# Four edits around the last batch and the head copies of a fused attention, mixing, Fourier and MLP kernel

## The chip, the cores and the metric

The kernel runs on one core of one Trainium2 chip. The metric is the device time of one launch in microseconds (us). Every product on TensorE is made of 32-bit numbers, most of them split into a high and a low half that TensorE multiplies separately.

## The reference

```python
# attention, batch 4, 8 heads, 576 positions, head width 64
scores = scale * q @ k.T
scores = where(scores >= max(scores) - tau, scores, -1e9)
attn = exp(scores - max); attn /= sum(attn) + 1e-9
x = (attn @ v) as (B, S, 512)
# mixing: xk, xr are x mixed with x one position earlier, by mu_k and mu_r
k = relu(xk @ w_k); v = (k * k) @ w_v; r = sigmoid(xr @ w_r)
x = r * v
# Fourier transform over positions and channels, then an MLP behind a layer norm
u = x + real(fft(fft(x, axis=1), axis=2))
mu = mean(u, -1); var = mean((u - mu) ** 2, -1)
un = (u - mu) / sqrt(var + 1e-6)
out = u + relu(un @ w_ch1) @ w_ch2
```

## The kernel before

The attention is cut into 144 tiles of up to 128 queries, 9 to a pair of heads and 36 to a batch. A slot n of the program works on several tiles at once: TensorE makes the scores of tile n (`qk`, line 816), transposes the probabilities of tile n-3 (line 832) and multiplies those of tile n-4 by v (`pv`, line 849); VectorE takes the row maximum of tile n (line 1350) and masks tile n-1 (line 1361); ScalarE takes the exponential of tile n (line 1092), copies the transposed probabilities of tile n-2 (line 1101) and, where a head ends with tile n-4, copies its output into `x_att`, divided by the row sums (`copy_head`, lines 1114 and 1119). For the first head of a pair that is four copies of 128x64 and two of 64x64 for the tail that both heads share; for the second head it is four copies.

The dense work of a batch (transposes of x, mixing, r, k, v, fold, the transforms y and u) is spread over the 36 slots of the next batch by tables of slots such as `MIX_AT` and `Y_AT`. Each engine has its own list of generators (`mixing`, `dense`), and `run_beside` moves them on once a slot. Every engine runs its instructions strictly in the order in which the program issues them, and waits on semaphores. The last batch (`alone(d)`) has no attention beside it: its dense work alone sets the time there. After it comes an MLP over 5 chunks of 464 columns (`mlp`, `chunk`), with the layer norm of the next chunk prepared beside the current one.

The norm of the first chunk is prepared within the dense work of the last batch. GpSimd adds the four channel tiles of u (`add_tiles`, lines 732 to 739: two sums, their sum, its high half, its low half), TensorE sums over partitions (`mean`, line 855, put behind the first product of stage v), VectorE subtracts the mean (`center`, line 1394), ScalarE squares (line 1261), GpSimd adds the tiles of the squares in the same way, and TensorE makes the variance (`variance`, line 855 again, behind the fourth product of stage v). In between GpSimd makes the low halves of the mixed inputs (`mix_l`, line 685).

The tables of the last transform lie in a scratch tensor in device memory, stored there in slot 34 of the first batch. Each batch loads them into `cs` behind its last product of stage v, the cosines (line 521) and then the sines (line 522), because `cs` shares its place with buffers of stage v. The u groups on TensorE wait for the cosines at g = 0 and for the sines at g = 1 (lines 1003 and 1005). The queue of SyncE issues them between loads of w_1. `u_in` holds two chunks of u; both are loaded early in the last batch.

At the start VectorE makes the high half of k and the low halves of q of the first head: for the first 128 queries (line 1329), then for the other 512 (line 1339). GpSimd makes the low halves of later heads (line 635).

## Time and profile before

| | us |
|---|---|
| median of 3 runs | 1079.55 (1079.39 to 1081.67) |
| the profiled execution | 1079.17 |
| its span | 1077.4 |
| TensorE busy with matmuls | 1053.3 (98%) |
| VectorE busy | 578.3 (54%) |
| ScalarE busy | 511.2 (47%) |
| GpSimd busy | 422.5 (39%) |

The span is the time from the first instruction to the last; the device time of the same execution is 1.8 us longer. Matmuls are pipelined: the profile lets one of 288 columns last 0.30 us, while the next starts 0.13 us after it. A stop of TensorE therefore shows in the starts of neighbouring matmuls, and less, or not at all, in the busy time.

### The profile page before, as it was taken

The page shows a single profiled execution, that of the slowest core. Times are in us where ns is not written, and L with a number is a line of the kernel's source. Part 1 is how long each engine was busy: PE and PEld are TensorE (multiplying, and loading weights), DVE is VectorE, ACT ScalarE, POOL GpSimd, SP SyncE. Part 2 cuts the span into 40 slices and gives each one's busy share as a digit, 9 for nine tenths or more (in the row PEclk, how much of TensorE's full clock was granted, in tenths as well). Part 3 has the DMA queues.
Part 4 walks back from the last instruction along what each step waited for, and adds up shares of the span by engine and source line. Part 5 has one row for each costly group of instructions (what it writes and reads, how often), then busy time and mean ns, then how long its engine had stood idle before and what let it go on. Part 6 is the DMA issues. An engine that isn't in the chain of part 4 may idle for free.

```text
span 1077.4 us, 18500 instructions
## 1 busy us (share of the span) xinstructions
PE 1053.3 (98%) x7088; PEld 1000.4 (93%) x7088; DVE 578.3 (54%) x1112; ACT 511.2 (47%) x1250; POOL 422.5 (39%) x371
## 2 busy tenths in 40 slices
PE   7999899999999999999999999999999999999998
PEld 6999899999999999999999988888888888888998
DVE  6888885467865467865455768344124124123211
ACT  5998775646775746775746553221111111111110
POOL 4878784343664333664322564341111111111000
PEclk9999999999999999999999999999999999999999
DMA  8635111024212024211014118200100100200000
GB/s 245 191 94 184 42 41 55 6 79 125 89 38 58 1 80 125 91 36 36 2 45 148 75 41 292 96 1 20 52 1 7 65 1 1 70 1 1 37 1 34
DMA packets 43800, 70.10 MB, mean 65 GB/s; under 512 B 4288, under 2 KB 25664, under 8 KB 43200
## 3 DMA queue, kind: packets, MB, share of 16 engines
q1 hardware_dynamic: 43408, 68.59, 20.3%
q8 instruction: 56, 0.92, 0.3%
q10 hardware_dynamic: 304, 0.33, 0.1%
q14 instruction: 32, 0.26, 0.1%
HBM read 56.50 MB, written 12.41 MB: 64 GB/s over the span
## 4 chain that ended last, share of the span: by engine, by line
PE 80%; DVE 6%; ACT 6%; POOL 4%; issue 3%; DMA 0%; DVEq 0%; SPq 0%; ACTq 0%; POOLq 0%
PE PB L789 20%; PE PB L791 20%; PE PB L790 20%; PE PB L849 9%; PE PB L816 6%; PE PB L832 5%; DVE probs L1361 2%; DVE neg_s L1350 1%; ACT probsT L1101 1%; ACT exps L1092 1%; ACT x_att L1114 1%; ACT mix_v L1163 1%; POOL wkl L651 1%; POOL q_hl L635 0%; POOL cs_lo L663 0%
## 5 line engine op out<-in xcount | busy, mean ns | idle before, releaser
L1307 ACT ACTIVATE h_hi<-PB 128x464 fp32r<-128x464 f32 (+1 forms) x80 | 44.5, 556 | 331.8 <-PE PB L791 331.8
L1565 DVE SCALAR_TENSOR_TENSOR h_lo<-PB,h_hi 128x464 fp32r<-128x464 f32 (+1 forms) x80 | 51.0, 638 | 257.8 <-ACT h_hi L1307 257.8
L849 PE MATMUL PB<-v_sb,probsT 128*128 128x64 f32 (+1 forms) x1440 | 177.5, 270 | 0.0
L849 PEld LDWEIGHTS PB<-v_sb,probsT 128*128 128x128 f32 x1440 | 172.1, 192 | 0.0
L1361 DVE SCALAR_TENSOR_TENSOR probs<-neg_s,thresh,exps 128x576 f32<-128x576 f32 x144 | 159.4, 1107 | 2.4 <-ACT exps L1092 2.3
L1101 ACT ACTIVATE probsT<-PB 128x384 f32<-128x384 f32 (+1 forms) x288 | 110.2, 437 | 72.6 <-PE PB L832 71.2
L1350 DVE TENSOR_SCALAR_CACHE_REDUCE neg_s<-PB,taus 128x576 f32<-128x576 f32 x144 | 117.0, 812 | 46.8 <-PE PB L816 43.4
L791 PE MATMUL PB<-un_h,w1l 128*128 128x464 f32 (+1 forms) x320 | 118.9, 371 | 0.0
L790 PE MATMUL PB<-h_lo,w2h 128*128 128x464 f32 (+1 forms) x320 | 118.8, 371 | 0.0
L789 PE MATMUL PB<-h_hi,w2h 128*128 128x464 f32 (+1 forms) x320 | 118.8, 371 | 0.0
L791 PE MATMUL PB<-h_hi,w2l 128*128 128x464 f32 (+1 forms) x320 | 118.8, 371 | 0.0
L789 PE MATMUL PB<-un_h,w1h 128*128 128x464 f32 (+1 forms) x320 | 118.7, 371 | 0.0
L790 PE MATMUL PB<-un_l,w1h 128*128 128x464 f32 (+1 forms) x320 | 118.6, 370 | 0.0
L1092 ACT ACTIVATE exps<-neg_s,negmax 128x576 f32<-128x576 f32 x144 | 111.6, 775 | 0.0
L685 POOL TENSOR_TENSOR mix_l<-mix_v,mix_h 128x288 fp32r<-128x288 f32 x64 | 56.0, 876 | 129.1 <-ACT mix_h L1178 128.4
L832 PE MATMUL PB<-ident,probs 128*128 128x128 f32 (+1 forms) x720 | 103.1, 274 | 2.0 <-ACT probsT L1101 1.3
L816 PE MATMUL PB<-k_hi,q_hl 128*128 128x288 f32 x320 | 75.3, 317 | 12.5 <-DVE q_hl L1329 7.1
L832 PEld LDWEIGHTS PB<-ident,probs 128*128 128x128 f32 (+1 forms) x720 | 81.7, 135 | 4.0 <-issue 2.8
L703 POOL TENSOR_TENSOR k_sql<-k_sq,k_sqh 128x288 fp32r<-128x288 f32 x56 | 48.8, 878 | 87.2 <-DVE k_sq L1450 87.2
L789 PE MATMUL PB<-k_sqh,wvh 128*128 128x288 f32 x256 | 78.5, 307 | 0.5 <-POOL k_sql L703 0.3
L789 PE MATMUL PB<-mix_h,wkh 128*128 128x288 f32 x256 | 78.2, 306 | 0.3 <-POOL mix_l L685 0.3
L1380 DVE SCALAR_TENSOR_TENSOR mix_v<-xT,mus,mix_v 128x288 f32<-128x288 f32 x64 | 51.5, 805 | 47.2 <-ACT mix_v L1163 47.0
(176 smaller groups left out, 2386.8 us busy)
## 6 DMA issues: line engine op xcount, KB each, us to landing
q_raw<-qT_dram SPq DMA_DIRECT2D x62, 160.0 KB, 3.1
k_raw<-kT_dram SPq DMA_DIRECT2D x64, 144.0 KB, 3.1
w_raw<-w_dram SPq DMA_DIRECT2D x8, 1024.0 KB, 9.2
cs<-cs_scr SPq DMA_DIRECT2D x8, 870.0 KB, 6.6
u_scr<-x2T SPq DMA_DIRECT2D x4, 1152.0 KB, 4.8
cd<-cd_scr SPq DMA_DIRECT2D x4, 1032.0 KB, 5.0
v_sb<-v_dram SPq DMA_DIRECT2D x16, 256.0 KB, 3.2
u_in<-u_scr SPq DMA_DIRECT2D x4, 928.0 KB, 5.9
```

The lines of the kernel that those rows point to most:

```text
L685: nc.gpsimd.tensor_tensor(mix_l[kind][:, dt, :], mix_v[:, i % 2, :], mix_h[kind][:, dt, :].bitcast(F32), ALU.subtract).then_inc(mixl_ready, 1)
L789: nc.tensor.matmul(o, ah, rh, start=start, stop=False)
L790: nc.tensor.matmul(o, ah, rl, start=False, stop=False)
L791: return nc.tensor.matmul(o, al, rh, start=False, stop=stop)
L816: last = nc.tensor.matmul(scores(n)[:, half, :], q_hl[:, h, i * P128:(i + 1) * P128], kk[:, h, half * HALF:half * HALF + HALF], start=h == ...
L832: last = nc.tensor.transpose(bank(4 + unit % 2)[0:keys, (kt - k0) * P128:(kt - k0 + 1) * P128], probs[:, n % 2, kt * P128:kt * P128 + keys ...
L849: last = nc.tensor.matmul(bank(6 + p)[:, i * DH:i * DH + width], probsT[:, n % 2, kt * P128:(kt + 1) * P128], v_sb[:, kt, pair % 2, p * DH ...
L1092: nc.scalar.activation(exps[:, n % 2, :], neg_s[:, n % 2, :], ACT.Exp, bias=negmax[:, col:col + 1], scale=-1.0).then_inc(exp_ready, 1)
L1101: nc.scalar.activation(probsT[:, n % 2, k0 * P128:k1 * P128], bank(4 + unit % 2)[:, 0:(k1 - k0) * P128], ACT.Copy).then_inc(unit_copied, 1)
L1350: nc.vector.tensor_scalar(neg_s[:, n % 2, :].rearrange("p (a n) -> p a n", a=2), scores(n), taus[:, 2:3], None, ALU.mult, ALU.min, accum_o ...
L1361: nc.vector.scalar_tensor_tensor(probs[:, n % 2, 0:S], neg_s[:, n % 2, :], thresh[:, col:col + 1], exps[:, n % 2, :], ALU.is_le, ALU.mult, ...
L1380: nc.vector.scalar_tensor_tensor(mix_v[:, i % 2, :], xT[:, dt, 1 + c * HALF:1 + (c + 1) * HALF], mus[:, kind, dt:dt + 1], mix_v[:, i % 2, ...
```

## The change

The first chunk's sums go from GpSimd to VectorE, with the rounding to the high half by ScalarE. A head's copies are issued in two slots: three of the four and then the fourth with the two tails for the first head of a pair, two and two for the second. The cosines of the last batch's transform get a place of their own, over the second half of `u_in`, and are loaded early in that batch; the second chunk of u is loaded when the transform is done. `cs` becomes two tensors, `cosines` and `sines`, and the scratch tensor is laid out the same way, so that each load is one contiguous run per partition, and the tables are stored by four copies in place of two. The low halves of the first head's other queries are made by GpSimd.

The parts of the diff follow the order of the program: places, SyncE, GpSimd, ScalarE (head copies, `round_first` in stage r of the last batch), VectorE.

```diff
-        cs = r.put("cs", [P128, 2, ST, 2 * FS], F32)
+        cosines = r.put("cosines", [P128, 2, ST, FS], F32)
+        sines = r.put("sines", [P128, 2, ST, FS], F32)
...
+        second = Place(r.at - DT * W * 4)
+        cosines_alone = second.put("cosines_alone", [P128, 2, ST, FS], F32)
...
+                def load_cosines(d):
+                    sp.dma_start(cosines_of(d)[:, :, :, :], cs_scr[:, 0]).then_inc(cs_in, 16)
...
                     sp.wait_ge(v_ready, d * 8 + 8)
-                    sp.dma_start(cs[:, :, :, 0:FS], cs_scr[:, :, :, 0:FS]).then_inc(cs_in, 16)
-                    sp.dma_start(cs[:, :, :, FS:2 * FS], cs_scr[:, :, :, FS:2 * FS]).then_inc(sines_in, 16)
+                    if not alone(d):
+                        load_cosines(d)
+                    sp.dma_start(sines[:, :, :, :], cs_scr[:, 1]).then_inc(sines_in, 16)
...
                         load_u(0, 0)
-                        load_u(1, 1)
+                        load_cosines(d)
                         load_w2(0)
                     yield u_at(d)[4] + 2
                     if d == B - 1:
                         load_w2(1)
                         sp.wait_ge(dft_ready, B * 5)
+                        load_u(1, 1)
                         load_w2(2)
...
+                pool.wait_ge(y_padded, 1)
+                pool.wait_ge(head0_q_hi, 2)
+                pool.wait_ge(head0_k_low, 1)
+                nc.gpsimd.tensor_tensor(q_hl[64:128, 0, P128:SQ], q_raw[64:128, 0, P128:SQ], q_hl[64:128, 0, P128:SQ].bitcast(F32), ALU.subtract).then_inc(qk_split, 1)
+                pool.wait_ge(qk_split, 1)
...
-                            nc.gpsimd.memset(mean512[:, :], 1.0 / D)
-                            sum_u(0, 0, 1)
-                        if stage == "v" and c == 0 and alone(d):
-                            yield 19
-                            sum_squares(0)
+                            nc.gpsimd.memset(mean512[:, :], 1.0 / D).then_inc(mean_set, 1)
...
-                def copy_head(n):
+                def copy_head(n, again):
...
+                    some = (3, FULL) if p == 0 else (2, FULL)
+                    for i in range(some[0], some[1]) if again else range(some[0]):
...
-                    if p == 0:
+                    if again and p == 0:
...
-                    last.then_inc(head_out, 1)
+                    if again:
+                        last.then_inc(head_out, 1)
...
+                                if alone(d) and c == 1 and dt == 0:
+                                    round_first(sums)
...
+                                if alone(d) and c == 1 and dt == 3:
+                                    round_first(sq_sums)
...
+                def round_first(done):
+                    act.wait_ge(done, 2)
+                    nc.scalar.activation(part_h[:, :], part[:, 0, :], ACT.Copy).then_inc(done, 1)
...
+                    for again in (False, True):
+                        done = n - 4 - again
+                        if 0 <= done < TILES and done % TILES_PAIR in (TAIL, TILES_PAIR - 1):
+                            copy_head(done, again)
...
-                dve.wait_ge(head0_q_hi, 2)
-                nc.vector.tensor_tensor(q_hl[64:128, 0, P128:SQ], q_raw[64:128, 0, P128:SQ], q_hl[64:128, 0, P128:SQ].bitcast(F32), ALU.subtract).then_inc(qk_split, 1)
...
+                def add_first_tiles(tiles, done):
+                    nc.vector.tensor_tensor(part[:, 0, :], tiles[:, 0, :], tiles[:, 1, :], ALU.add)
+                    nc.vector.tensor_tensor(part[:, 1, :], tiles[:, 2, :], tiles[:, 3, :], ALU.add).then_inc(done, 1)
+                    dve.wait_ge(done, 1)
+                    nc.vector.tensor_tensor(part[:, 0, :], part[:, 0, :], part[:, 1, :], ALU.add).then_inc(done, 1)
+                def low_of_first(done):
+                    dve.wait_ge(done, 3)
+                    nc.vector.tensor_tensor(part_l[:, :], part[:, 0, :], part_h[:, :].bitcast(F32), ALU.subtract).then_inc(done, 1)
...
+                            yield 17
+                            dve.wait_ge(u_loaded[0], 16)
+                            add_first_tiles(u_in[:, 0], sums)
+                            low_of_first(sums)
                             yield 18
                             center(0, 0)
+                            dve.wait_ge(sq_ready, 1)
+                            add_first_tiles(sqr[0], sq_sums)
+                            yield 19
+                            low_of_first(sq_sums)
```

## Rows read from the trace of the kernel before

**Rows 1.** The page's first part: busy time, share of the span, instructions.

```profile
PE 1053.3 (98%) x7088; PEld 1000.4 (93%) x7088; DVE 578.3 (54%) x1112; ACT 511.2 (47%) x1250; POOL 422.5 (39%) x371
```

**Rows 2.** Windows: stretch, length, busy time per engine, clock, DMA share, GB/s.

```profile
36.00:54.00 18.00, 17.36 (x143) 16.38 (x142) 13.82 (x33) 17.94 (x46) 16.62 (x13) 1.00 0.61 185
```

**Rows 3.** Waits of TensorE: who waited for whom, total us, times, longest.

```profile
PE PB L816 <- DVE neg_s L1350: 4.9, 10, 1.2
```

**Rows 4.** Timeline of the last batch: start, duration, engine, line, operation, idle before.

```profile
619.72 1.76 ACT L1261 ACTIVATE sqr<-cent 128x1856 f32<-128x1856 f32 x1 [4.89 <-DVE cent L1394]
...
622.65 1.41 POOL L732 TENSOR_TENSOR part<-sqr 128x464 f32<-128x464 f32 x1
...
626.94 0.29 PE L791 MATMUL PB<-k_sqh,wvl 128*128 128x288 f32 x1
628.55 0.48 PE L855 MATMUL PB<-part_h,mean 128*128 128x464 f32 x1 [1.32 <-POOL part_l L739]
...
637.11 0.64 DVE L1416 TENSOR_TENSOR rstd<-rstd,newt 128x464 f32<-128x464 f32 x1
```

**Rows 5.** Timeline around the mean of the first chunk.

```profile
609.59 1.45 DVE L1450 TENSOR_TENSOR k_sq<-k_relu 128x288 f32<-128x288 f32 x1
...
614.64 0.88 DVE L1459 TENSOR_TENSOR k_sql<-k_sq,k_sqh 128x288 fp32r<-128x288 f32 x1
...
616.98 0.37 PE L855 MATMUL PB<-part_h,mean 128*128 128x464 f32 x1
```

**Rows 6.** Timeline around the last transform: the queue of SyncE, VectorE, TensorE.

```profile
656.20 0.54 SPq L521 DMA_DIRECT2D cs<-cs_scr  x1
656.78 0.65 SPq L522 DMA_DIRECT2D cs<-cs_scr  x1
...
660.27 2.20 DVE L1494 TENSOR_TENSOR y_l<-PB,y_h 128x258 fp32r<-128x258 f32 x6 [1.69 <-ACT y_h L1241]
...
661.33 0.28 PE L791 MATMUL PB<-cd,fold_l 128*33 128x258 f32 x1
662.20 0.37 PE L789 MATMUL PB<-cs,y_h 128*128 128x290 f32 x1 [0.60 <-DVE y_l L1494]
...
663.34 0.30 PE L791 MATMUL PB<-cs,y_l 128*128 128x290 f32 x1
664.46 0.37 PE L789 MATMUL PB<-cs,y_h 128*128 128x290 f32 x1 [0.82 <-issue]
```

**Rows 7.** Timeline of slots 3 to 5 behind the first batch.

```profile
264.36 0.93 ACT L1114 ACTIVATE x_att<-PB,rowinv 128x64 f32<-128x64 f32 x4
...
266.93 0.73 DVE L1380 SCALAR_TENSOR_TENSOR mix_v<-xT,mus,mix_v 128x288 f32<-128x288 f32 x1 [1.50 <-ACT mix_v L1163]
...
268.31 0.46 PE L936 MATMUL PB<-ident,x_att 64*128 64x64 f32 x4 [0.40 <-DVE xT L1437]
269.05 0.53 PE L816 MATMUL PB<-k_hi,q_hl 128*128 128x288 f32 x2 [0.27 <-DVE neg_s L1350]
```

**Rows 8.** Timeline at two other head copies of the same batch.

```profile
250.32 0.39 PE L789 MATMUL PB<-cd,fold_h 128*128 128x258 f32 x1
...
283.58 0.93 ACT L1114 ACTIVATE x_att<-PB,rowinv 128x64 f32<-128x64 f32 x4
...
288.32 0.40 PE L816 MATMUL PB<-k_hi,q_hl 128*128 128x288 f32 x1
```

**Rows 9.** Timeline of the start.

```profile
8.03 0.69 DVE L1339 TENSOR_TENSOR q_hl<-q_raw,q_hl 64x512 fp32r<-64x512 f32 x1
...
9.42 0.68 PE L816 MATMUL PB<-k_lo,q_hl 128*128 128x288 f32 x2
...
10.60 1.56 POOL L635 TENSOR_TENSOR q_hl<-q_raw,q_hl 64x640 fp32r<-64x640 f32 x1
...
10.88 1.89 DVE L1361 SCALAR_TENSOR_TENSOR probs<-neg_s,thresh,exps 128x576 f32<-128x576 f32 x1
...
18.38 0.43 PE L816 MATMUL PB<-k_lo,q_hl 128*128 128x288 f32 x2
```

More of the change, by code:

```diff
@@ L365, in build @@
         u_in = r.put("u_in", [P128, 2, DT, W], F32)
+        second = Place(r.at - DT * W * 4)
+        cosines_alone = second.put("cosines_alone", [P128, 2, ST, FS], F32)
+        assert second.at <= r.at
         early = Place(r.at)
@@ L456, in build @@
         u_loaded = [sem("u_loaded0"), sem("u_loaded1")]
-        sums, sq_sums = sem("sums"), sem("sq_sums")
+        sums, sq_sums, mean_set = sem("sums"), sem("sq_sums"), sem("mean_set")
         mean_ready, cent_ready, sq_ready, var_ready = [sem(n) for n in ("mean_r", "cent_r", "sq_r", "var_r")]
@@ L466, in slot_before, with cosines_of @@
             return ft - 2 if ft >= 3 else {0: 15, 1: 13, 2: 14}[ft] - MFT + 1
+        def cosines_of(d):
+            return cosines_alone if alone(d) else cosines
         def gate_of(d, c):
@@ L588, in _ @@
                         sp.dma_start(cd_scr[:, 1], cd_lo[:, :, :].bitcast(F32)).then_inc(tables_stored, 16)
-                        sp.dma_start(cs_scr[:, 0], cs_hi[:, :, :].bitcast(F32)).then_inc(tables_stored, 16)
-                        sp.dma_start(cs_scr[:, 1], cs_lo[:, :, :].bitcast(F32)).then_inc(tables_stored, 16)
+                        for kind in range(2):
+                            cols = slice(kind * FS, (kind + 1) * FS)
+                            sp.dma_start(cs_scr[:, kind, 0], cs_hi[:, :, cols].bitcast(F32)).then_inc(tables_stored, 16)
+                            sp.dma_start(cs_scr[:, kind, 1], cs_lo[:, :, cols].bitcast(F32)).then_inc(tables_stored, 16)
                         sp.dma_start(odd_scr, odd_r[:, :].bitcast(F32)).then_inc(tables_stored, 16)
@@ L1101, in copy_units @@
                         nc.scalar.activation(probsT[:, n % 2, k0 * P128:k1 * P128], bank(4 + unit % 2)[:, 0:(k1 - k0) * P128], ACT.Copy).then_inc(unit_copied, 1)
-                def copy_head(n):
+                def copy_head(n, again):
                     p, pair = half_of(n), n // TILES_PAIR
-                    act.wait_ge(pv_ready, n + 1)
-                    act.wait_ge(inv_ready, pair * 2 + p + 1)
-                    if pair >= PAIRS:
-                        act.wait_ge(tx_ready, pair // PAIRS * 5)
+                    if not again:
+                        act.wait_ge(pv_ready, n + 1)
+                        act.wait_ge(inv_ready, pair * 2 + p + 1)
+                        if pair >= PAIRS:
+                            act.wait_ge(tx_ready, pair // PAIRS * 5)
                     col = pair % PAIRS * 2 * DH + p * DH
-                    for i in range(FULL):
+                    some = (3, FULL) if p == 0 else (2, FULL)
+                    for i in range(some[0], some[1]) if again else range(some[0]):
                         t = i + p * QT
```

18 lines of the change are left out of this document (9 added, 9 removed).

## The prediction, made before the changed kernel ran

> **What bounds the kernel.** Read the page's first part first: TensorE is busy for 1053.3 us [rows 1], so 24.1 us of the span are idle. That is the most an edit off TensorE could win if busy time were exact. It isn't: a matmul of 288 columns lasts 0.30 us in the profile while its successor starts 0.13 us later, so each stop loses up to 0.16 us more than the idle column shows. I therefore take every stop from starts: the distance to the next start, minus the usual one (0.13 us for 288 columns, 0.11 us for one of `pv`). Next come TensorE's waits, which put 4.9 us in ten pieces on the row maxima [rows 3], and then the timelines at the places that the change touches. The chunks of the MLP, from 670 us on, show no wait of TensorE at all, so nothing after that point wins or loses as long as its inputs come in time.
>
> **Part 1: the first chunk's sums.** TensorE's last product of stage v starts at 626.94, the next matmul would be due at 627.07, and the variance starts at 628.55, waiting for GpSimd's last sum: a stop of 1.48 us [rows 4]. Behind the squares, which end at 619.72 + 1.76 = 621.48, GpSimd spends five operations, the first of 1.41 us [rows 4]. Now VectorE does three sums, ScalarE one rounding, VectorE one subtraction. The trace has no such sum on VectorE; the nearest row is a product of two SBUF tiles of the same 464 columns, 0.64 us [rows 4]. So: 3 x 0.64, 0.56 for the rounding (the same copy in the page's h_hi group), 0.64, and some 0.9 for the mixing step that now stands in VectorE's queue between them: 621.48 + 4.0 = 625.5, or 1.6 us before 627.07. The upper bound is GpSimd's own 1.41 us per operation: 621.48 + 4 x 1.41 + 0.56 + 0.9 = 628.6, which wins nothing. I take 0.64 because GpSimd, the engine that slows VectorE here, has lost its ten operations. Gain 1.48 us.
>
> The sums of u itself must not come late. TensorE takes the mean at 616.98 without a stop [rows 5]. VectorE can start them only behind the last low half of stage k, which ends at 614.64 + 0.88 = 615.5 [rows 5]. If that stayed, 3 x 0.64 + 0.56 + 0.64 gives 618.6 and a stop of 1.6 us. But six operations of 288 columns between 607 and 615.5 last 0.88 to 1.45 us where the same ones take 0.45 a little earlier; the first and last of the slow ones that matter are in [rows 5]. GpSimd's sums of u run through exactly this stretch and now go. Their excess is 4.7 us in all, so the low half ends at about 610.8 and the sums at about 614. ScalarE stands in its rounding until then, with the second gate and the next mixing step behind it; both ran at 613.2 to 614.8 already. No cost.
>
> After the variance comes a chain on VectorE (reciprocal, Newton step, scaling) with products of stage k between, and TensorE then stops three times for `k_sql`, about 1.0 us together. That chain starts from the variance, so it moves with it, and the 1.0 us stay.
>
> **Part 2: the cosines ahead.** The last y matmul starts at 661.33 and the next is due at 661.45; the first u matmul starts at 662.20, a stop of 0.75. Group g = 1 starts at 664.46 where 663.47 was due, a stop of 0.99 [rows 6]. The view names y_l for the first. But the first y_l is done at about 660.7, one sixth into its six [rows 6], and it is all that this matmul needs of them. So the cosines, issued at 656.20, must have landed last, 5.9 us later; the second stop has no engine as releaser and is the sines. After the change the sines are alone in front, issued at 656.20 instead of 656.78. At the cosines' 5.9 us they land at 662.1; g = 1 wants them at 661.45 + 9 x 0.133 = 662.65. Both stops go: 1.74 us. Bounds: if the sines still took the 7.6 us that they take now they would land at 663.8 and cost 1.1 of it back, leaving 0.6; nothing more than 1.74 is there. What is late next is y_l, which trails y by two operations, and not on this path. The load of `u_in` moved behind the transform is first wanted by GpSimd after its last sum of the transform, several us later.
>
> **Part 3: head copies in two slots.** A second head's copies take 0.8 us of ScalarE (four starts in the 0.93), a first head's 1.45 with the two tails. Three places of a middle batch show them on the path.
> Slot 3: copies at 264.36; behind them ScalarE's mixing step releases VectorE at 266.93, which then copies x and takes the row maximum; TensorE stops at 268.31 (due 267.74) and 269.05 (due 268.64), together 0.98 [rows 7]. Half the copies moved away makes all this 0.4 us earlier. The transposes that need the whole head then start about 0.27 us later than now, but they stand in front of the first stop, which swallows it. Gain 0.4.
> Slot 35: the same engine reaches its y copy late behind 1.45 us of head copies; 250.32 stands where 250.05 was due [rows 8]. Of the copies 0.8 moves away. Gain 0.27.
> Slot 8: copies at 283.58, the stop ahead of 288.32 is 0.25 (due 288.07) [rows 8], and another of 0.33 follows a slot later. The second half of the copies (0.83 us) falls between the two, where ScalarE has 0.76 idle. I take half of 0.4.
> That is 0.87 per batch, twice; the first batch has the places of slots 3 and 8 (0.6), the last neither, as its stops there come from other waits. Sum 2.3. Bounds: 0, if the moved copies delay the next slot as much; 4.9, the whole of [rows 3].
> Ahead of 60 us splitting gives nothing: ScalarE is busy for 17.94 of 18 us there [rows 2], and moving work by a slot inside a full stretch leaves its end where it was.
>
> **Part 4: the start.** VectorE loses 0.69 us between its set-up and the first row maximum [rows 9]; the scores are ready only at about 8.65, so the maximum gains 0.1. GpSimd needs about 1.3 for it (1.56 for 640 columns [rows 9]) from 7.8 on, so tile 1 may begin at 9.1 instead of 8.78. The first mask, at 10.88, lasts 1.89 us instead of its usual 0.81, and ends 0.6 after GpSimd's subtraction of the second head, 10.60 + 1.56 [rows 9]: the end of that subtraction decides, not when the mask could start, and it moves by 0.1 at most. Cost 0.1; bounds -0.1 (the maximum's gain) and +0.4 (all of tile 1's delay kept).
> The Trainium skill, "SBUF — State Buffer", Who interferes with whom, says that a VectorE instruction with two SBUF inputs and a GpSimd one that reads SBUF exclude each other for the whole instruction. By that the set-up's `max` of two columns would wait for the moved subtraction until 9.1, and the first row maximum, and ScalarE's first exponential with it, would come 0.4 us later than now instead of 0.1 earlier; the mask would still wait for the next subtraction, so the sum stays within the bound of +0.4. The trace agrees in the 1.89 us.
>
> **Sum.** -1.48 - 1.74 - 2.3 + 0.1 = -5.4 on the profiled execution's 1079.17, or 1073.8. The median of the runs is 0.4 higher, so the median after should be about 1074.2.
>
> **The rivals.**
> (a) The head copies win nothing: each stop comes back a slot later, because ScalarE's moved part is in front of the next exponential. For it: slot 8's numbers above, 0.83 against 0.76. Against it: in slots 3 and 35 ScalarE waits 0.4 to 1.5 us in the next slot. Time: 1079.55 - 3.1 = 1076.4.
> (b) The transfer bounds part 2: w_1 stands right behind the sines, and the 870 KB of cosines less in front change little. For it: the second load took 1.7 us longer than the first. Against it: the first had both behind it and took 5.9. The sines land at 663.8, part 2 gains 0.6, the rest stays: 1075.3.
> (c) The sums come late. VectorE's operations at 607 to 615 stay slow, the mean costs 1.6 us and part 1 nets zero: 1079.55 - 3.9 = 1075.7.
> (d) Slower than before. TensorE starts at its lower level: matmuls of 288 columns start 0.24 us apart in the first slots and 0.13 after 18 us [rows 9], 1.2 against 2.4 GHz, with 1.00 granted throughout. GpSimd's later half opens a gap of 0.4 us between tile 0 and tile 1. If the rise came later for it, each slot at the low level would cost up to 1.9 us (2.2 us of matmuls at double the distance). Four slots more, up to 27 us, would eat the 5.4 and end at 1081.8. Below three slots it only eats gain. Against it: the engine had gaps of 0.3 to 0.9 us there already.
>
> **How the numbers follow.** Forecast 0.55 with its own range 1073 to 1075.6; (a) 0.17; (b) 0.10; (c) 0.08; (d) 0.02; better than forecast, where all of slot 8 and the first batch's stops follow (1072.5) 0.05; and 0.03 for mixtures that leave less than 2 us. The range that leaves out 0.2 is 1072.4 to 1077.0. A difference of 0.2% is 2.2 us, about what runs of this kernel can tell from none. Forecast, (a), (b), (c) are all beyond it: faster 0.88, but cases together and noise reach it, which I put at same 0.09, slower 0.03.
>
> **What would show it.** Right: no idle time ahead of the variance on line 855's successor; the first u group 0.12 us behind the last y matmul and g = 1 right behind g = 0; VectorE's operations in 608 to 615 back at 0.45; the stops of slot 3 shorter by 0.4. Wrong: a wait of the mean on VectorE's low half; a wait at g = 1 that is no engine's; stops of 0.4 or more one slot behind the head copies; matmuls still 0.24 us apart beyond 20 us.

## The result and the profile after

| | before | after |
|---|---|---|
| median, us | 1079.47 (1078.79 to 1081.67, 4 runs) | 1071.68 (1071.40 to 1072.66, 4 runs) |
| profiled execution, us | 1079.17 | 1072.66 |
| its span, us | 1077.4 | 1070.9 |
| ratio | | 0.9926, 95% interval 0.9909 to 0.9943 |

The kernel is faster by 7.8 us. The forecast was 1074.2 with a range from 1072.4 to 1077.0, so the sign was right and the time lies 0.7 us below the range. Chance put the slowest of the four executions of the kernel after under the profiler: between the two traces the difference is 6.5 us, and 1.0 us more between the runs. Both parts are explained below.

The page's first part after, which answers to [rows 1], and TensorE's waits, which answer to [rows 3]:

```profile
PE 1051.8 (98%) x7088; PEld 1000.9 (93%) x7088; DVE 577.4 (54%) x1119; ACT 513.3 (48%) x1252; POOL 414.1 (39%) x362
```

```profile
PE PB L834 <- DVE neg_s L1381: 3.1, 4, 1.2
...
PE PB L951 <- ACT x_att L1136: 0.7, 3, 0.2
```

TensorE's busy time falls by only 1.5 us though the span falls by 6.5: the busy column is no measure of what an edit wins here. The waits on row maxima fall from ten, 4.9 us, to four, 3.1 us, and a new, smaller one on the head's second half (`x_att`) appears.

The instrument that explains the rest is a comparison of starts. Both traces hold the same 7088 matmuls in the same order; the start of each in one trace minus its start in the other is the offset, and it changes only where time is won or lost. From before to after it is -0.09 at the first matmul, +0.59 at 18 us, +0.53 at 50, -0.56 at 134, -1.24 at 269, -1.74 at 292, -2.43 at 430, -2.94 at 453 and -3.09 at 612; then -4.59 at the variance, -4.65 at the last y matmul, -5.40 at the first u group, -6.46 at the second, and -6.51 at the end. So the sums won 1.50, the cosines 1.87, the head copies 3.6, and the start cost 0.5.

The timeline of the last batch after, which answers to [rows 4, 5]:

```profile
608.09 0.63 DVE L1456 TENSOR_TENSOR part<-u_in 128x464 f32<-128x464 f32 x1
...
618.39 0.64 DVE L1456 TENSOR_TENSOR part<-sqr 128x464 f32<-128x464 f32 x1 [1.82 <-ACT sqr L1288]
618.77 0.93 POOL L707 TENSOR_TENSOR mix_l<-mix_v,mix_h 128x288 fp32r<-128x288 f32 x1 [6.85 <-ACT mix_h L1201]
618.95 1.25 DVE L1457 TENSOR_TENSOR part<-sqr 128x464 f32<-128x464 f32 x1
```

```profile
613.73 0.30 PE L809 MATMUL PB<-k_sqh,wvl 128*128 128x288 f32 x1
613.86 0.37 PE L873 MATMUL PB<-part_h,mean 128*128 128x464 f32 x1
...
623.82 0.29 PE L809 MATMUL PB<-k_sqh,wvl 128*128 128x288 f32 x1
623.96 0.37 PE L873 MATMUL PB<-part_h,mean 128*128 128x464 f32 x1
```

A sum takes 0.64 us on VectorE, as forecast. One takes 1.25, with GpSimd's `mix_l` beside it. The mean and the variance start 0.13 us behind the product ahead of them: no stop is left.

The transform after, with SyncE's queue, which answers to [rows 6]:

```profile
651.56 0.34 SPq L534 DMA_DIRECT2D sines<-cs_scr  x1
```

```profile
656.68 0.28 PE L809 MATMUL PB<-cd,fold_l 128*33 128x258 f32 x1
656.80 0.30 PE L807 MATMUL PB<-cosines_alone,y_h 128*128 128x290 f32 x1
...
657.88 0.29 PE L809 MATMUL PB<-cosines_alone,y_l 128*128 128x290 f32 x1
658.01 0.30 PE L807 MATMUL PB<-sines,y_h 128*128 128x290 f32 x1
```

Both stops are gone. The sines landed 5.7 us after their issue (657.3) where 5.9 was forecast, 0.7 us before they are wanted.

Slot 3, which answers to [rows 7]: the copies ahead of the mixing step are two in place of four, and VectorE's step ends its wait 0.4 us earlier (1.10 in place of 1.50).

```profile
263.52 0.53 ACT L1136 ACTIVATE x_att<-PB,rowinv 128x64 f32<-128x64 f32 x2
...
265.69 0.73 DVE L1411 SCALAR_TENSOR_TENSOR mix_v<-xT,mus,mix_v 128x288 f32<-128x288 f32 x1 [1.10 <-ACT mix_v L1186]
```

The two slots behind the first head of a pair, which answer to [rows 8]:

```profile
282.34 0.73 ACT L1136 ACTIVATE x_att<-PB,rowinv 128x64 f32<-128x64 f32 x3
...
285.57 0.31 ACT L1136 ACTIVATE x_att<-PB,rowinv 128x64 f32<-128x64 f32 x1
285.77 0.63 ACT L1141 ACTIVATE x_att<-PB,rowinv 64x64 f32<-64x64 f32 x2
286.82 0.43 PE L834 MATMUL PB<-k_hi,q_hl 128*128 128x288 f32 x2
```

The start, which answers to [rows 9]:

```profile
7.83 1.27 POOL L638 TENSOR_TENSOR q_hl<-q_raw,q_hl 64x512 fp32r<-64x512 f32 x1 [6.07 <-DVE k_lo L1364]
...
9.15 0.85 PE L834 MATMUL PB<-k_hi,q_hl 128*128 128x288 f32 x2 [0.59 <-POOL q_hl L638]
...
11.26 1.54 DVE L1392 SCALAR_TENSOR_TENSOR probs<-neg_s,thresh,exps 128x576 f32<-128x576 f32 x1
...
12.87 1.33 PE L850 MATMUL PB<-ident,probs 128*128 128x128 f32 x5
...
15.73 0.68 PE L834 MATMUL PB<-k_lo,q_hl 128*128 128x288 f32 x2
```

GpSimd's subtraction takes 1.27 us (1.3 forecast), tile 1 starts at 9.15 (9.1 forecast), and the first transposes at 12.87 against 12.84 before. The offset of this trace arises later, from +0.03 at 16.6 us to +0.59 at 18.0: the products of `pv` still start 0.21 us apart there, where those of the kernel before already start 0.11 us apart.

### The profile page after: what moved, and what is told of

It reads as the page before. It is cut to its first block, busy times and chain, and to the rows that moved or that the text cites. A ratio compares the mean times of both kernels' runs of the same rounds, so it can differ in the third digit from the quotient of the medians.

```text
span 1070.9 us, 18505 instructions
## 1 busy us (share of the span) xinstructions
PE 1051.8 (98%) x7088; PEld 1000.9 (93%) x7088; DVE 577.4 (54%) x1119; ACT 513.3 (48%) x1252; POOL 414.1 (39%) x362
## 4 chain that ended last, share of the span: by engine, by line
PE 89%; POOL 4%; ACT 3%; DVE 2%; issue 1%; DMA 0%; SPq 0%; DVEq 0%; ACTq 0%; POOLq 0%
PE PB L807 22%; PE PB L809 21%; PE PB L808 21%; PE PB L867 11%; PE PB L834 7%; PE PB L850 6%; ACT probsT L1121 1%; ACT exps L1112 1%; POOL wkl L673 1%; DVE probs L1392 1%; POOL cs_lo L685 0%; POOL k_lo L664 0%; DVE neg_s L1381 0%; POOL q_hl L657 0%; DMA k_raw<-kT_dram 0%
## 5 line engine op out<-in xcount | busy, mean ns | idle before, releaser
L809 PE MATMUL PB<-k_sqh,wvl 128*128 128x288 f32 x256 | 76.2, 298 | 0.0
```

Source lines behind the costliest of these rows:

```text
L809: return nc.tensor.matmul(o, al, rh, start=False, stop=stop)
```

## The experiments

All compare with the kernel before, run on the same chip beside them, and, by offsets, with a second trace of the kernel after, `a0_after_again`. Medians of the kernel before in the four groups: 1079.07 (a), 1078.62 (b, c1), 1078.80 (d), 1079.05 (e, c2). The groups ran on four chips; `a0_after_again` ran with group a alone.

### Each edit undone

`a0_after_again` is the kernel after, unchanged.

> The changed kernel once more, unaltered: the traced execution was 6.5 us shorter than that of before, the medians differ by 7.8. Theory S (the four edits add up to the 6.5 us of the trace, the rest is which execution was traced): 1072.0, 7.2 us under before with an interval that holds 6.5, and a trace in which TensorE's matmuls in the first slots have sped up by 17 us, with an offset of about 0 and not +0.5 us from there on. Rival X (something that the trace of after does not show wins another 1.3 us): 1071.7 or less again, with the same offset of +0.5 us at 20 us.

`a1_undo_q` gives the low halves of the first head's other queries back to VectorE:

```diff
-                nc.gpsimd.tensor_tensor(q_hl[64:128, 0, P128:SQ], q_raw[64:128, 0, P128:SQ], q_hl[64:128, 0, P128:SQ].bitcast(F32), ALU.subtract).then_inc(qk_split, 1)
...
+                nc.vector.tensor_tensor(q_hl[64:128, 0, P128:SQ], q_raw[64:128, 0, P128:SQ], q_hl[64:128, 0, P128:SQ].bitcast(F32), ALU.subtract).then_inc(qk_split, 1)
```

> The low halves of the first head's other queries are made by VectorE again, the other three edits stay. Theory S (VectorE's 0.69 us were not what the first mask waited for, and GpSimd's longer operation opens a gap on TensorE): 0 to 0.5 us faster than the changed kernel, 1071.2 to 1071.7, tile 1's scores again 0.4 us earlier and matmuls at the fast distance by about 16.8 us. Rival X (this edit is where the untraced 1.3 us come from): 1.0 to 1.3 us slower, 1072.7 to 1073.0.

`a2_undo_cosines` loads the cosines behind stage v again, in the new layout, and the second chunk of u early:

```diff
-            return cosines_alone if alone(d) else cosines
+            return cosines
...
-                    if not alone(d):
-                        load_cosines(d)
+                    load_cosines(d)
...
-                        load_cosines(d)
+                        load_u(1, 1)
...
-                        load_u(1, 1)
```

> Cosines and sines are both loaded behind the last product of stage v again, and the second chunk of u early; the new contiguous layout stays. Theory S (the two stops at the last transform were the two transfers): 1.75 us slower than the changed kernel, 1073.4, with stops of about 0.75 ahead of g = 0 and 1.0 ahead of g = 1. Rival L (the layout does part of it: one long run per partition lands sooner): the first stop is at most 0.3 us and the second under 0.6, so 0.3 to 0.9 us slower, 1072.0 to 1072.6.

`a3_undo_sums` gives the first chunk's sums back to GpSimd:

```diff
+                            sum_u(0, 0, 1)
...
+                            sum_squares(0)
...
-                                    round_first(sums)
...
-                                    round_first(sq_sums)
...
-                            add_first_tiles(u_in[:, 0], sums)
-                            low_of_first(sums)
...
-                            add_first_tiles(sqr[0], sq_sums)
-                            low_of_first(sq_sums)
```

> The first chunk's sums are GpSimd's again, the other three edits stay. Theory S: the stop of 1.48 us ahead of the variance is back and nothing else, so 1.5 us slower than the changed kernel, 1073.2. Rival V (VectorE, free of GpSimd's sums, wins more behind the variance or at the k_sql stops): 2 us slower or more, 1073.7 and up.

`b1_undo_heads` issues both parts of a head's copies in one slot:

```diff
-                            copy_head(done, again)
+                            if half_of(done) not in (0, 1):
+                                copy_head(done, again)
+                            elif not again:
+                                copy_head(done, False)
+                                copy_head(done, True)
```

> All head copies of a head are issued in one slot again, the other three edits stay. Theory S (the stops behind head copies of all batches go, as the trace of after shows: 1.2 us in each middle batch, some 1.2 in the first, 0.15 in the last): 3.7 us slower than the changed kernel, 1075.4. Rival F (the forecast's 2.3 us, with half of slot 8 and little in the first batch): 1074.0. Rival A (nothing, the copies only move a stop by a slot): 1071.7.

Medians and ratios: a0 1071.40 (0.9925, 0.9913 to 0.9937), a1 1071.89 (0.9930, 0.9918 to 0.9942), a2 1073.35 (0.9946, 0.9933 to 0.9958), a3 1073.16 (0.9943, 0.9931 to 0.9956), b1 1074.86 (0.9965, 0.9952 to 0.9979). Against 1071.4 the edits cost 0.5, 1.95, 1.8 and 3.5 us to undo, 7.7 together, which is the whole difference. That it fits so closely is partly luck: b1 ran on another chip, where the kernel before was 0.45 us faster (3.9 with that taken out), and the six executions of a2 lie 3.6 us apart. The traces are the better evidence.

a0 fits neither reading that was recorded for it. Its median is 0.6 us below theory S's 1072.0, and its offset against the kernel before is -1.16 at 18.5 us, where S had 0 and X +0.5.

The offsets against a0, at times of a0:

| us | 18.5 | 50 | 99 | 110 | 136 | 252 | 275 | 292 | 411 | 433 | 452 | 630 | 662 |
|---|---|---|---|---|---|---|---|---|---|---|---|---|---|
| after | 1.74 | 1.22 | 1.19 | 1.22 | 1.26 | 1.26 | 1.27 | 1.26 | 1.26 | 1.27 | 1.26 | 1.12 | 1.20 |
| a1 | 1.05 | 0.45 | 0.41 | 0.43 | 0.43 | 0.45 | 0.44 | 0.47 | 0.47 | 0.46 | 0.48 | 0.35 | 0.41 |
| a2 | 0.39 | -0.20 | -0.23 | -0.19 | -0.17 | -0.17 | -0.17 | -0.16 | -0.16 | -0.16 | -0.15 | -0.10 | 3.85 |
| a3 | 1.67 | 1.34 | 1.35 | 1.35 | 1.34 | 1.36 | 1.35 | 1.38 | 1.38 | 1.37 | 1.39 | 2.88 | 2.95 |
| b1 | 0.15 | -0.30 | -0.15 | 0.00 | 0.83 | 1.12 | 1.53 | 2.03 | 2.34 | 2.75 | 3.25 | 3.31 | 3.37 |

Two traces of the same kernel (the first line) differ by 1.74 us at 18.5 and stay 1.1 to 1.3 apart from 50 us on. Every other edit shows as steps at its own place: the sums 1.5 to 1.6 between 610 and 630 us, the head copies 3.7 in eleven steps of 0.1 to 0.7 from 107 to 449 us and 0.1 behind them, so rival (a) of the prediction falls. Here is the sum's place in `a3_undo_sums`, the stop of before back:

```profile
624.00 0.29 PE L813 MATMUL PB<-k_sqh,wvl 128*128 128x288 f32 x1
625.60 0.48 PE L877 MATMUL PB<-part_h,mean 128*128 128x464 f32 x1 [1.31 <-POOL part_l L761]
```

### What the early cosines do

`a2_undo_cosines` loses 3.9 us in its trace at one place, twice the stops of [rows 6]. Its timeline, then its windows (columns as in [rows 2]):

```profile
650.35 0.34 SPq L518 DMA_DIRECT2D cosines<-cs_scr  x1
650.73 1.73 SPq L533 DMA_DIRECT2D sines<-cs_scr  x1
...
655.59 0.30 PE L805 MATMUL PB<-cosines,y_h 128*128 128x290 f32 x1
...
656.66 0.29 PE L807 MATMUL PB<-cosines,y_l 128*128 128x290 f32 x1
659.12 0.58 PE L805 MATMUL PB<-sines,y_h 128*128 128x290 f32 x1 [2.17 <-issue]
659.50 0.45 PE L806 MATMUL PB<-sines,y_h 128*128 128x290 f32 x1
```

```profile
655.00:658.00 3.00, 1.96 (x16) 1.69 (x14) 2.98 (x6) 1.17 (x4) 3.00 (x1) 1.00 0.93 329
658.00:662.00 4.00, 2.88 (x12) 2.91 (x13) 3.97 (x2) 0.33 (x1) 0.63 (x1) 0.62 1.05 402
```

The first stop is gone though the cosines stand behind v: in one contiguous run they take 4.8 us, not 5.9. The sines take 8.3 and stop TensorE for 2.33 us. Behind that stop the granted clock is 0.62 in the mean of the stretch, the matmuls start 0.24 us apart, and that costs 1.5 us more (the offset is 2.32 at the stop's end and 3.84 where the spacing is 0.13 again, at 662.4). The six executions run from 1071.7 to 1075.3; that the faster ones had no such drop is likely, but only this one has a trace. So the price of this edit is read from the stops of [rows 6] and their absence in the kernel after, not from a2.

`c1_heads_alone` is the kernel before with split head copies and the new layout, `c2_q_alone` with GpSimd's subtraction at the start and the new layout:

```diff
-                    sp.dma_start(cs[:, :, :, 0:FS], cs_scr[:, :, :, 0:FS]).then_inc(cs_in, 16)
-                    sp.dma_start(cs[:, :, :, FS:2 * FS], cs_scr[:, :, :, FS:2 * FS]).then_inc(sines_in, 16)
+                    load_cosines(d)
+                    sp.dma_start(sines[:, :, :, :], cs_scr[:, 1]).then_inc(sines_in, 16)
```

> The kernel before with the head copies in two slots and the contiguous table layout, and none of the other three edits. Theory S (gains add up): 3.7 us under the kernel before, 1075.8. Rival F: 2.3 us under it, 1077.2. Rival Y (the edits need each other): under 1.5 us.

> The kernel before with only two things of the change: GpSimd makes the low halves of the first head's other queries, and the tables of the transform are stored and loaded in the new layout (cosines still behind stage v). With the layout the first stop of the transform goes and the second grows by as much, so it counts nothing. Prediction: tile 1 begins 0.3 to 0.4 us later, the first transposes within 0.1 us: 1079.2, no difference. Rival one: the lighter VectorE lets TensorE rise to its fast spacing earlier, as the difference of two medians (1071.4 against 1071.9) could be read: 1078.3. Rival two: the gap ahead of tile 1 makes it rise later, 1079.9.

c1: 1074.91 (0.9963, 0.9951 to 0.9976), an offset of -4.1 us at the end. c2: 1077.94 (0.9989, 0.9980 to 0.9997). The transform in `c2_q_alone`:

```profile
661.03 0.30 PE L809 MATMUL PB<-cosines,y_h 128*128 128x290 f32 x1
...
663.98 0.37 PE L809 MATMUL PB<-sines,y_h 128*128 128x290 f32 x1 [1.58 <-issue]
```

With the layout alone the first stop goes and the second grows: 1.76 us in c2 and 1.62 in c1, against 0.75 and 0.99, 1.74 together, before. The layout is worth nothing by itself. What wins is that 870 KB no longer stand in front of the sines, and rival (b) falls: they took 7.6 to 8.3 us behind the cosines and 4.5 to 5.7 alone (5.7 in the trace of the kernel after, 4.5 to 5.6 in the other twelve with the early cosines).

The trace of before also has the landing of the cosines by itself (`--dma --window 656:656.6`): 656.20 + 5.91 = 662.11, 0.09 us ahead of the first u matmul.

```profile
cs<-cs_scr SPq DMA_DIRECT2D x1, 870.0 KB, 5.9
```

### Where the head copies win

`b2_undo_first_heads` and `b3_undo_second_heads` undo the split for one head of each pair, the other three for places (`whole` says which heads are copied in one slot; the conditions of b2 and b3 are written here in the form of the others):

```diff
+                            whole = half_of(done) == 0                                   # b2
+                            whole = half_of(done) == 1                                   # b3
+                            whole = done < 31                                            # e1
+                            whole = done % TILES_BATCH == TAIL and done >= TILES_BATCH   # e2
+                            whole = done % TILES_BATCH in (31, 35)                       # e3
```

> Only the first head of each pair (four copies and two tails, 1.45 us) is copied in one slot again; the second heads stay split. Theory S: slots 35 and 8 of the middle batches (0.35 + 0.5 each) and slot 8 of the first (0.7 us at 130 to 135 us) are lost: 2.4 us slower than the changed kernel, 1074.1. Rival: the two kinds count alike by their length, two thirds of the whole, 1074.0 to 1074.2 but with the loss at the start of the program, too. The trace tells them apart: by S the offset up to 100 us is that of the changed kernel.

> Only the second head of each pair (four copies, 0.8 us) is copied in one slot again. Theory S: slot 3 of the three inner batches (0.4 us each) is lost: 1.2 us slower than the changed kernel, 1072.9, and together with the run for the first heads this makes up the loss of the run with both undone. Rival: the splits overlap, either alone wins most, and this one costs 0.3 or less.

> The kernel after with the head copies of the first 31 tiles (all ahead of 75 us) issued in one slot again. In the kernel with no split at all TensorE was 0.3 us ahead at 43 to 56 us and 0.4 us at 100 us. Theory (splitting inside ScalarE's full stretch wins nothing and delays it a little): TensorE at 100 us is 0.2 to 0.4 us earlier and about that reaches the end, 1071.0 to 1071.2. Rival, the prediction's 'nothing': within 0.1 us at 100 us, 1071.4. Second rival: what is ahead at 100 us is lost in the stop at 107 us, where it was 0.00 in the kernel with no split, and the end is the same.

> The kernel after with only the slot-8 head copies (the first head of the first pair) of the second, third and fourth batch in one slot again. The prediction took this place at 0.2 us a batch. Theory: both stops behind it come back whole, 0.25 and 0.25 us, in two batches, and 0.8 us in the one at 128 to 133 us: TensorE's last start moves by +1.6 to +1.9 us against the kernel after, 1073.0 to 1073.3. Rival, the prediction's size: +0.4 to +0.6 us, 1071.9.

> The kernel after with only the head copies of slots 35 and 3 of each batch in one slot again. Prediction: 0.27 and 0.4 us in each of two middle batches, and 0.4 in the first: +1.7 us, 1073.1. Theory from the kernels with one head undone: 0.27 and 0.43 a batch, the same, +1.6 to +1.8. Rival: the two places overlap with slot 8's, so that three parts undone one at a time sum to clearly more than the 3.4 us of all at once.

Medians: b2 1075.02 (0.9960, 0.9947 to 0.9972), b3 1072.92 (0.9945, 0.9933 to 0.9958), e1 1072.74 (0.9937, 0.9925 to 0.9950), e2 1073.15 (0.9948, 0.9934 to 0.9961), e3 1073.16 (0.9947, 0.9935 to 0.9960). Offsets against a0, at times of a0:

| us | 18.5 | 50 | 99 | 110 | 136 | 252 | 275 | 292 | 411 | 433 | 452 | 662 | behind 50 |
|---|---|---|---|---|---|---|---|---|---|---|---|---|---|
| b2 | 1.54 | 1.07 | 1.22 | 0.98 | 1.82 | 2.14 | 2.13 | 2.64 | 2.96 | 2.95 | 3.43 | 3.55 | 2.5 |
| b3 | 0.63 | 0.07 | 0.05 | 0.49 | 0.48 | 0.50 | 0.91 | 0.93 | 0.95 | 1.35 | 1.37 | 1.49 | 1.4 |
| e1 | 0.28 | -0.17 | -0.17 | -0.14 | -0.14 | -0.14 | -0.15 | -0.13 | -0.11 | -0.12 | -0.09 | -0.19 | 0.0 |
| e2 | 0.33 | -0.25 | -0.29 | -0.24 | 0.58 | 0.60 | 0.59 | 1.09 | 1.13 | 1.12 | 1.61 | 1.59 | 1.8 |
| e3 | -0.16 | -0.46 | -0.32 | -0.16 | -0.12 | 0.19 | 0.60 | 0.62 | 0.92 | 1.34 | 1.35 | 1.47 | 1.9 |

The copies ahead of 75 us are worth nothing in the trace, as the prediction said of those ahead of 60; my theory, that their split costs 0.3 us, falls in it. e1's median is 1.3 us above a0's, its executions lie at 1071.3 to 1071.6 and at 1072.7 to 1073.2, and the profiled one is the fastest, 1071.28: the slower ones have no trace, and why there are two groups stays open. By medians alone one would misread this set: b2's lies above b1's, though b1 undoes more, because b2's execution carries 1.1 us from the start. The other two places make up all of it, and three partial undoings, 0.0, 1.8 and 1.9, give b1's 3.7.

The rival of overlapping places falls with this sum. Slot 8 is the term that was mis-sized, in the first batch most of all. There the trace of before had a stop of 0.61 us that the prediction did not read (due 129.53); it is back in e2 and gone in a0:

```profile
130.14 0.53 PE L816 MATMUL PB<-k_hi,q_hl 128*128 128x288 f32 x2 [0.45 <-DVE neg_s L1350]
```

The same slot in a middle batch, in `e2_slot8_whole`:

```profile
283.14 0.29 ACT L1111 ACTIVATE thresh<-negmax,taus 128x1 f32<-128x1 f32 x1
...
286.40 0.29 ACT L1111 ACTIVATE thresh<-negmax,taus 128x1 f32<-128x1 f32 x1 [0.75 <-DVE neg_s L1386]
286.43 0.54 PE L834 MATMUL PB<-k_hi,q_hl 128*128 128x288 f32 x2
```

and the kernel after again at the same place:

```profile
282.05 0.29 ACT L1111 ACTIVATE thresh<-negmax,taus 128x1 f32<-128x1 f32 x1 [0.25 <-DVE neg_s L1381]
...
284.31 0.31 ACT L1136 ACTIVATE x_att<-PB,rowinv 128x64 f32<-128x64 f32 x1
...
284.51 0.63 ACT L1141 ACTIVATE x_att<-PB,rowinv 64x64 f32<-64x64 f32 x2
...
285.32 0.30 ACT L1111 ACTIVATE thresh<-negmax,taus 128x1 f32<-128x1 f32 x1 [0.18 <-DVE neg_s L1381]
...
285.58 0.43 PE L834 MATMUL PB<-k_hi,q_hl 128*128 128x288 f32 x2
```

ScalarE waits 0.75 us for the row maximum where the copies are whole. With the moved part in front of it, 284.31 to 285.14, it still waits 0.18. The slot has not become longer: its two `thresh` operations are 3.26 us apart in e2 and 3.27 in a0. The moved part is 0.83 us from its first start to its last end, but it takes only 0.57 of the idle time: it overlaps the copy of the probabilities in front of it by 0.11, and that copy itself starts 1.63 us behind the first `thresh` in place of 1.75. So ScalarE is not late for the row maximum, and this one comes 0.5 us earlier against the surroundings, because the threshold and the mixing step of the slot before no longer stand behind 0.83 us of copies. The stop of TensorE behind it goes.

### The start, and when TensorE becomes fast

Three kernels ask whether the differences that arise by 18.5 us are TensorE's level, that is, whether its 288-column matmuls start 0.24 us apart (1.2 GHz) or 0.13 (2.4 GHz). 18 matmuls of zeros are put where it waits for the first inputs (`d1_warm` on the kernel after, `d2_warm_undo_q` with the start's edit undone, `d3_warm_before` on the kernel before):

```diff
+                pe.wait_ge(y_padded, 1)
+                for i in range(18):
+                    nc.tensor.matmul(bank(3)[:, 0:288], y_h[ST - 1][:, 0:P128], y_l[ST - 1][:, 0:288], start=True, stop=True)
                 pe.wait_ge(ident_loaded, 16)
```

> The kernel after, with 18 matmuls of zeros (288 columns each, result overwritten later) put on TensorE between about 1.9 and 6.2 us, where it only waits for the first inputs. Theory (the spread of about 1 us between executions, and the 1 to 1.7 us by which single profiles differ at 18 us, come from when TensorE leaves the 0.24 us spacing): the scores of tiles 0 to 4 run at 0.13 us, the offset at 18 us against the first execution of after is -1.7 or more, of which about 1.2 is left behind the ScalarE-bound stretch, so 1070.3 to 1071.0, and the runs lie within 0.6 us of each other. Rival (the start is set by the inputs and by VectorE's and ScalarE's chain, the spacing does not matter): 1071.4 with the spread unchanged. A second rival, that zeros do not bring the rise: the spacing at tile 0 is still 0.24 us, 1071.4.

> As the run before, with the same 18 matmuls, and the low halves of the first head's other queries by VectorE again. With the clock level taken out of it this gives the price of that edit. Theory: tile 1 begins 0.4 to 0.5 us earlier than with GpSimd, but the first transposes wait for the first mask and begin within 0.1 us, so the end is within 0.2 us of the run before. Rival: the earlier start of tile 1 carries through to the first transpose and wins 0.4 us.

> The kernel before with the same 18 matmuls of zeros. Theory: its profiled execution already had the rise at about 16.7 us, so it wins about as much as the kernel after does, 0.5 to 1.2 us: 1077.9 to 1078.6, and the ratio of the two kernels with the matmuls is that of the four edits without the start: about -7.2 us. Rival: no change, 1079.1.

d1: 1072.41 (0.9939, 0.9927 to 0.9951). d2: 1072.16, 1070.6 to 1077.5 (0.9950, 0.9935 to 0.9965). d3: 1078.78, 1077.3 to 1085.5 (1.0007, 0.9992 to 1.0022). My theory of a gain falls by the medians: none of the three is faster than its own kernel without the matmuls. Five of d3's twelve executions lie at 1077.3 to 1077.9, though, where three of the 21 of the kernel before beside them lie (1077.7 to 1077.8); whether the matmuls win in executions in which nothing goes wrong behind them stays open, as none of those has a trace. Its premise holds. The windows of `d1_warm`:

```profile
7.00:9.00 2.00, 1.03 (x4) 0.58 (x4) 1.50 (x5) 0.00 (x0) 1.17 (x1) 1.00 1.12 227
9.00:12.00 3.00, 2.85 (x12) 2.47 (x12) 2.16 (x5) 1.93 (x4) 2.83 (x4) 0.62 0.51 128
12.00:15.00 3.00, 2.42 (x11) 1.76 (x9) 2.75 (x7) 1.21 (x3) 1.98 (x2) 0.50 0.96 258
```

The zeros do bring the fast level to tile 0, but TensorE waits there for its inputs, and after these waits the granted clock falls to 0.50, from 9.7 to 16.6 us in its record. Its offset against a0 is +1.08 at 18.5 us and +0.77 at the end. The profiled execution of `d3_warm_before`, 1085.17 us, is one of the two slowest:

```profile
11.36 0.76 PE L832 MATMUL PB<-ident,probs 128*128 128x128 f32 x5 [0.27 <-DVE probs L1364]
14.62 0.85 PE L816 MATMUL PB<-k_hi,q_hl 128*128 128x288 f32 x2 [2.50 <-POOL k_lo L642]
```

```profile
12.00:15.00 3.00, 0.50 (x3) 0.38 (x2) 2.87 (x7) 2.30 (x6) 2.49 (x2) 0.80 0.90 242
15.00:20.00 5.00, 5.00 (x24) 4.95 (x24) 1.95 (x6) 1.92 (x5) 2.84 (x3) 0.50 0.81 247
```

A faster start reaches GpSimd's `k_lo` 2.5 us too early, TensorE stops for it, and then runs at half its clock until 27.4 us, some 13 us. (0.5 us of the 2.5 are GpSimd's own: its subtraction ahead of `k_lo` took 2.15 us where it takes 1.56 in [rows 9], with the mask started 0.06 us before it.) Against the kernel before it is 1.6 us ahead at 13 us, 0.5 behind at the end of the stop and 5.4 behind from 22 us on; 0.6 more comes at the last transform, where the cosines and sines landed 6.1 and 8.4 us after their issue: 6.0 at the end. So rival (d) described a real mechanism with the right price, a slot of 4.16 us in place of 2.20, set off by another stop.

As to the start's edit: with the level moved in both, d2 ends 0.2 us ahead of d1 in the traces and by the medians, nothing that could be told from no difference. On its own (c2) the median was 1.1 us lower, with an interval just below 1, though the profiled execution, one of its slower ones, is only 0.4 us ahead in its span. Undone (a1) it was 0.5 higher, within the spread. TensorE's rise, in the traces without added matmuls, tells how that can be. Each of these fifteen traces has its first record of the granted clock, a step to 1.00, at the point where the spacing changes, and the later it comes, the later the whole rest is:

| first record, us | traces | offset against a0 at 50 us |
|---|---|---|
| 12.4 to 13.9 | a0, a2, b1, e2, e3 | -0.46 to 0.00 |
| 15.1 to 15.5 | b3, c2, d4, e1 | -0.17 to 0.19 |
| 16.1 to 16.7 | before, a1, c1 | 0.19 to 0.68 |
| 17.6 to 17.9 | after, a3, b2 | 1.08 to 1.35 |

The offset follows the rise, whichever engine makes the low halves. The second group of `pv` starts at 18.8 to 19.2 us in the three kernels with VectorE's subtraction (before, a1, c1). In those with GpSimd's it starts at 17.9 to 18.7 in nine of twelve traces and at 19.6 to 19.8 in three, the first trace of the kernel after among them. `c2_q_alone`, whose rise is recorded at 15.2 us:

```profile
14.34 0.85 PE L836 MATMUL PB<-k_hi,q_hl 128*128 128x288 f32 x2
14.99 0.53 PE L836 MATMUL PB<-k_lo,q_hl 128*128 128x288 f32 x2
15.35 0.43 PE L836 MATMUL PB<-k_hi,q_hl 128*128 128x288 f32 x2
```

That the edit brings the rise forward is suggested, not shown: only three traces stand on one side, and three of the twelve on the other rise later than all of those.

### A version that could have been faster

In the kernel after the transposes of x wait for the head's second half three times (266.86, and 0.24 idle there, is one). `d4_last_head_ahead` puts those copies ahead of the copy of the probabilities in that slot:

```diff
+                    ahead = 0 <= n - 5 < TILES and (n - 5) % TILES_BATCH == TILES_BATCH - 1
+                    if ahead:
+                        copy_head(n - 5, True)
                     if 0 <= n - 2 < TILES:
                         copy_units(n - 2)
...
-                        if 0 <= done < TILES and done % TILES_PAIR in (TAIL, TILES_PAIR - 1):
+                        if 0 <= done < TILES and done % TILES_PAIR in (TAIL, TILES_PAIR - 1) and not (again and ahead):
```

> The kernel after; in the first slot 4 of each batch, ScalarE makes the second half of the last head's copies ahead of its copy of the transposed probabilities, not behind it. In the kernel after, the transposes of x stop TensorE for up to 0.4 us there (at 107.7, 266.9 and 426.9) and wait for these copies, which start 0.63 us behind the copy of the probabilities. Theory: each stop shrinks by 0.2 to 0.4 us, 0.6 to 1.1 us over three batches: 1070.4 to 1070.9. Rival: the copy of the probabilities, 0.5 us later, holds up the next slot's transposes or pv, and nothing is won: 1071.4 or up to 0.5 us more.

1071.37 (0.9929, 0.9917 to 0.9941): no gain. The transposes start 0.38 us earlier against their surroundings in each of the three places, and the scores behind them are where they were: the row maximum is what TensorE waits for next. Nothing run here beats the kernel after.

## Why the forecast was right or wrong, point by point

**Part 1** was right in place and size: 1.50 us in the two traces, 1.5 in a3, against 1.48. The sums of u are not late: VectorE's slow operations at 607 to 615 became fast when GpSimd left, and rival (c) falls. The 1.25 us of one sum shows that GpSimd's `mix_l` still slows it; three of 0.64 were an optimistic sum. That the whole came out (3.8 us from the squares to the low half against 4.0) is partly luck: the 0.6 us too little there were met by the mixing step, put at 0.9, which VectorE made in 0.51 while ScalarE rounded.

**Part 2** was right: 1.87 against 1.74. The 0.13 more is the slow restart behind each stop (a first matmul of 0.37 us and 0.2 to the next). The argument that the first stop was the cosines and not `y_l`, against what the view named, is confirmed by the landing at 662.11 and by c1 and c2: with `y_l` as it was, the shorter transfer took the stop away.

**Part 3** is the step that failed, in size only: 2.3 forecast, 3.6 in the traces. Slot 35 was taken at 0.27 and measured 0.31 (e3), slot 3 at 0.40 and 0.41. Slot 8 was "half of 0.4" and is 0.50 in each middle batch (e2). The first batch was 0.6 and is 0.31 at slot 3 and 0.82 at slot 8, and 0.1 us lies in the last batch. For the middle batches the mistake was in one comparison: the moved 0.83 us was held against the 0.76 us that ScalarE idles in the kernel before, as if it took all of its length. It took 0.57 of the idle time, ScalarE still waited 0.18, and 0.50 of the two stops named at [rows 8], 0.58 together, went. For the first batch slot 8 was sized after the middle ones, at 0.2, while its own stop of 0.61 at 130.14 stood in the trace of before. The case in which all of it follows was in the prediction, at 1072.5 and a chance of 0.05. "Ahead of 60 us splitting gives nothing" was right in the trace of e1; e1's median, 1.3 us above a0's, leaves it unproven.

**Part 4** had the steps right, but not what decides the term, the level of TensorE behind them: +0.1 forecast; +0.5 in the first pair of traces, -0.5 and -1.1 by the medians of a1 and c2. The set-up's `max` of two columns took 0.16 us; it had started at 7.75, before GpSimd's instruction at 7.83, so the Trainium skill's rule of "SBUF — State Buffer", Who interferes with whom, was not put to the test there. It was for the mask: 1.54 us beside GpSimd's subtraction, ending 0.6 us behind it, where the rule and the trace agree but for 0.2 us (the mask alone takes 0.81).

**The range** was too narrow at its lower end for two reasons. (The profiled execution, 1072.66, lies 1.1 us below the 1073.8 forecast for it.) The head copies' upper case had too small a chance, and no term of the sum stood for the moment at which TensorE's clock rises in the first 20 us, which moves single executions of one kernel by 1.2 us at the end (after against a0) and which the profile before showed in [rows 9]. I had it as a rival on the slow side only. Of the 2.5 us between 1074.2 and 1071.7 the head copies are 1.3 and the cosines 0.1; the start took 0.4 more in the trace than forecast; 1.0 is the profiled execution of after above its own median, and 0.4 is what I had added because that of before lay below its own.

## What to carry to other kernels

Where a piece of work moves to the next slot, don't hold its full length against the idle time there: 0.83 us of small operations took 0.57 us of it, because they overlap their neighbours. Ask instead what ends that idle time, and whether it moves with the work ahead of it. Read each batch's own stops, too, before sizing one after another. Before believing a difference of 1 us between two versions, compare the starts of the same matmuls in both traces: an edit's effect is a step at its own place, while a difference made in the first 20 us is carried to the end, and two traces of one kernel here differ by 1.2 us in that way. Work that only makes an engine arrive earlier at a wait can cost much more than it wins, if the wait makes TensorE's clock fall.

## What the runs showed of the hardware that was not expected

- A stop of TensorE of 2.3 us in the last batch (`a2_undo_cosines`), and one of 2.5 at the start (`d3_warm_before`), were followed by a stretch with matmuls 0.24 us apart, the 1.2 GHz level: 3.4 us with 1.5 us lost, and 13 us with 4.9 lost. The stops of 1.5 to 1.8 us in c1, c2 and a3 were followed by none.
- At the start TensorE has the 0.24 us spacing up to 12 to 18 us while the views print a granted clock of 1.00. The trace has no record of the clock there: its first one is the step to 1.00 where the spacing changes (17.93 us in the trace of the kernel after, 12.89 in a0). In `d1_warm`, where TensorE had first been fast, the same spacing stands beside 0.50. At the start, read the level from the spacing.
- Where VectorE and GpSimd overlapped, the operation that started second was the one drawn out. In the kernel after the mask starts 0.6 us behind GpSimd's subtraction (10.64, 1.55 us) and takes 1.54 us in place of 0.81; in `d3_warm_before` it starts 0.06 us ahead of the subtraction and takes 0.82, and the subtraction takes 2.15.
- A table of 870 KB, the first of its pair in the queue, took 5.9 and 6.1 us to land (two traces) when each partition's part was in six pieces of 1160 bytes, and 4.7 to 4.9 (three traces) as one contiguous run, though the time of both tables together did not fall. One contiguous table alone took 4.5 to 5.7.
